# Gate and value products of a gated MLP as seven block products on tiles of 1024 tokens, with all attention scores ahead of the tiles

## Chip, cores and metric

The kernel runs on one core of one Trainium2 chip. The metric is the device time of one execution in microseconds; lower is better. Times of the kernel before are the median, lowest and highest of 3 runs, and one more execution was profiled.

## The reference

Everything is float32. The attention works over channels, the MLP over tokens.

```
B, N, C = 2, 6016, 256            # q, k, v: [B, N, C];  d_ff = 1536
qn = q / (norm(q, axis=1) + 1e-6);  kn = k / (norm(k, axis=1) + 1e-6)
s  = kn.transpose(0, 2, 1) @ qn / tau                 # [B, 256, 256]
a  = exp(s - max(s, -1));  a /= a.sum(-1) + 1e-9
x  = (v @ a).reshape(12032, 256)                      # tokens
xn = x / sqrt(mean(x * x, -1) + 1e-6) * rms_g
g  = xn @ w_gate;  val = xn @ w_val                   # [12032, 1536]
out = (g * sigmoid(g) * val) @ w_out                  # [12032, 256]
```

## The kernel before

**Arithmetic.** For precision every float32 operand of a large product is split in a high part (`_hi`, rounded by ScalarE to the matmul's format) and a low part (`_lo`, the rest, by VectorE), and a product is three matmuls: high by high, high by low, low by high (`product`, L382). So each 128x128 weight block costs three matmuls over a tile's columns. The scores of the first batch are made from unsplit float32 instead (`raw_scores`, L391).

**Stages.** A group is four chunks of 128 tokens of q and k (12 groups a batch, one of three chunks). SP loads groups into a ring of three buffers; TensorE makes the scores, ScalarE squares q and k for the norms, VectorE adds the squares up. All 12 groups of batch 0 and four of batch 1 pass so ahead of the tiles. Norms, softmax and the split of `a` follow for batch 0. The other eight groups of batch 1 pass during the first eight tiles, split in high and low (`scores1`, L404).

A tile is 512 tokens (12 a batch, one of 384). Of the next tile, v is loaded and turned by VectorE (`turn_v`), split (`vt`), multiplied with `a` (`attend`, L435), scaled by the inverse root of its mean square (`x_rms`, `x_scale`), passed through DRAM by SP (`pass_x`, L313), turned (`turn_x`) and split (`xt`), all between the units of the current tile.

**A unit** is one of 12 slices of 128 of d_ff. `gate_val` (L458) makes the gate (2 weight blocks, 6 matmuls, bank `ps_gate`) and the value (6 more, `ps_val`). ScalarE makes silu (L632), VectorE the product with the value (L882), ScalarE its high part (L636), VectorE its low part (L887). `project` (L470) then adds 2 blocks of 3 matmuls to the output banks `ps_out`, one unit behind:

```
gate_val(t, odd, f, n)
project(t, f - 1, n)
```

The units use two buffers in turn: TensorE waits for `hid_done` of two units ago before a gate and for `hid_split` before a projection. After unit 11 VectorE turns `ps_out` to `stage` (L1009) and SP stores it. The order on each engine is written out by hand in `step`. GpSimd only makes two constants.

## Time and profile before

| | us |
|---|---|
| median of 3 runs | 1343.12 (1339.2 to 1345.58) |
| profiled execution, own time | 1343.76 |
| its span | 1342.0 |
| TensorE busy | 1317.4 (98%), 6224 matmul records |
| VectorE busy | 701.6 (52%), 1294 instructions |
| ScalarE busy | 529.0 (39%), 1008 instructions |
| GpSimd busy | 0.8 (0%), 7 instructions |
| moved by DMA | 78.10 MB, mean 58 GB/s |
| mean granted TensorE clock | 0.992 |

The span is the profiled window on the core; the own time is what that execution took, 1.76 us more. The profile calls TensorE PE, VectorE DVE, ScalarE ACT, GpSimd POOL and SyncE SP. A busy time counts the instructions' own time only; matmuls overlap, so the mean of one is longer than the pace at which they follow each other, and the pace is what sums to time.

### The profile page before, as it was taken

The page shows a single profiled execution, that of the slowest core. Times are in us where ns is not written, and L with a number is a line of the kernel's source. Part 1 is how long each engine was busy: PE and PEld are TensorE (multiplying, and loading weights), DVE is VectorE, ACT ScalarE, POOL GpSimd, SP SyncE. Part 2 cuts the span into 40 slices and gives each one's busy share as a digit, 9 for nine tenths or more (in the row PEclk, how much of TensorE's full clock was granted, in tenths as well). Part 3 has the DMA queues.
Part 4 walks back from the last instruction along what each step waited for, and adds up shares of the span by engine and source line. Part 5 has one row for each costly group of instructions (what it writes and reads, how often), then busy time and mean ns, then how long its engine had stood idle before and what let it go on. Part 6 is the DMA issues. An engine that isn't in the chain of part 4 may idle for free.

```text
span 1342.0 us, 17895 instructions
## 1 busy us (share of the span) xinstructions
PE 1317.4 (98%) x6224; PEld 1117.1 (83%) x6224; DVE 701.6 (52%) x1294; ACT 529.0 (39%) x1008; POOL 0.8 (0%) x7
## 2 busy tenths in 40 slices
PE   8889999999999999999999999999999999999998
PEld 7768888888888888888888888888888888888887
DVE  4775555555555555455454455454454454454453
ACT  5564434344344343333343333333333333333332
POOL 0000000000000000000000000000000000000000
PEclk9899999999999999999999999999999999999999
DMA  8851212312223112111112111121121121121010
GB/s 295 274 153 47 63 32 72 84 31 63 50 68 70 31 31 63 32 28 46 42 32 55 36 32 36 43 46 31 32 62 31 31 63 31 31 59 32 16 40 12
DMA packets 171192, 78.10 MB, mean 58 GB/s; under 512 B 148626, under 2 KB 165010, under 8 KB 171154
## 3 DMA queue, kind: packets, MB, share of 16 engines
q1 hardware_dynamic: 171154, 77.62, 22.2%
q8 instruction: 21, 0.34, 0.1%
q14 instruction: 17, 0.14, 0.0%
HBM read 53.48 MB, written 24.12 MB: 58 GB/s over the span
## 4 chain that ended last, share of the span: by engine, by line
PE 94%; DVE 2%; DMA 2%; ACT 1%; issue 1%; SPq 0%; DVEq 0%; ACTq 0%
PE ps_out L387 28%; PE ps_gate L387 28%; PE ps_val L387 28%; PE ps_aux L387 7%; PE ps_aux L396 2%; DMA raw<-in_k_dram 1%; PE ps_out L396 1%; DVE hid L882 0%; ACT hid_hi L636 0%; DMA xn<-x_rows 0%; DVE hid_lo L887 0%; DMA x_rows<-xn 0%; DVE stage L1009 0%; DVE wo_lo L915 0%; ACT s_acc L585 0%
## 5 line engine op out<-in xcount | busy, mean ns | idle before, releaser
L882 DVE TENSOR_TENSOR hid<-ps_val,sg 128x512 f32<-128x512 f32 (+1 forms) x288 | 195.4, 679 | 349.5 <-PE ps_val L387 335.3
L636 ACT ACTIVATE hid_hi<-hid 128x512 fp32r<-128x512 f32 (+1 forms) x288 | 179.6, 624 | 457.5 <-DVE hid L882 457.5
L887 DVE TENSOR_TENSOR hid_lo<-hid,hid_hi 128x512 fp32r<-128x512 f32 (+1 forms) x288 | 196.2, 681 | 201.9 <-ACT hid_hi L636 201.9
L632 ACT ACTIVATE sg<-ps_gate 128x512 f32<-128x512 f32 (+1 forms) x288 | 169.8, 590 | 248.3 <-PE ps_gate L387 247.8
L387 PE MATMUL ps_out<-hid_hi,wo_hi 128*128 128x512 f32 (+1 forms) x576 | 222.8, 387 | 4.7 <-DVE hid_lo L887 4.3
L387 PE MATMUL ps_gate<-xt_hi,wgv_hi 128*128 128x512 f32 (+1 forms) x576 | 222.9, 387 | 2.1 <-DVE xt_lo L873 2.1
L387 PE MATMUL ps_gate<-xt_lo,wgv_hi 128*128 128x512 f32 (+1 forms) x576 | 222.2, 386 | 0.0
L387 PE MATMUL ps_out<-hid_hi,wo_lo 128*128 128x512 f32 (+1 forms) x576 | 222.0, 385 | 0.0
L387 PE MATMUL ps_out<-hid_lo,wo_hi 128*128 128x512 f32 (+1 forms) x576 | 221.8, 385 | 0.0
L387 PE MATMUL ps_gate<-xt_hi,wgv_lo 128*128 128x512 f32 (+1 forms) x576 | 221.8, 385 | 0.0
L387 PE MATMUL ps_val<-xt_hi,wgv_lo 128*128 128x512 f32 (+1 forms) x576 | 221.5, 384 | 0.0
L387 PE MATMUL ps_val<-xt_lo,wgv_hi 128*128 128x512 f32 (+1 forms) x576 | 221.5, 384 | 0.0
L387 PE MATMUL ps_val<-xt_hi,wgv_hi 128*128 128x512 f32 (+1 forms) x576 | 221.4, 384 | 0.0
L387 PEld LDWEIGHTS ps_out<-hid_hi,wo_hi 128*128 128x128 f32 x576 | 108.2, 188 | 29.0 <-DVE hid_lo L887 7.8
L387 PEld LDWEIGHTS ps_gate<-xt_hi,wgv_hi 128*128 128x128 f32 x576 | 108.4, 188 | 23.1 <-issue 2.1
L387 PEld LDWEIGHTS ps_gate<-xt_hi,wgv_lo 128*128 128x128 f32 x576 | 108.4, 188 | 21.0
L387 PEld LDWEIGHTS ps_out<-hid_hi,wo_lo 128*128 128x128 f32 x576 | 108.3, 188 | 20.7
L387 PEld LDWEIGHTS ps_val<-xt_hi,wgv_hi 128*128 128x128 f32 x576 | 108.1, 188 | 20.7
L387 PEld LDWEIGHTS ps_val<-xt_lo,wgv_hi 128*128 128x128 f32 x576 | 108.1, 188 | 20.7
L387 PEld LDWEIGHTS ps_val<-xt_hi,wgv_lo 128*128 128x128 f32 x576 | 108.1, 188 | 20.5
L387 PEld LDWEIGHTS ps_out<-hid_lo,wo_hi 128*128 128x128 f32 x576 | 108.3, 188 | 20.3
L387 PEld LDWEIGHTS ps_gate<-xt_lo,wgv_hi 128*128 128x128 f32 x576 | 108.5, 188 | 19.6
(100 smaller groups left out, 1030.6 us busy)
## 6 DMA issues: line engine op xcount, KB each, us to landing
v_in<-in_v_dram SPq DMA_DIRECT2D x88, 128.0 KB, 3.1
out_dram<-stage SPq DMA_DIRECT2D x88, 128.0 KB, 2.4
raw<-in_q_dram SPq DMA_DIRECT2D x21, 512.0 KB, 4.2
raw<-in_k_dram SPq DMA_DIRECT2D x21, 512.0 KB, 5.3
x_rows<-xn SPq DMA_DIRECT2D x21, 512.0 KB, 2.9
xn<-x_rows SPq DMA_DIRECT2D x84, 128.0 KB, 2.8
stage<-in_moe_w_out_dram SPq DMA_DIRECT2D x6, 256.0 KB, 3.2
raw<-in_q_dram SPq DMA_DIRECT2D x3, 384.0 KB, 4.6
```

What stands on the lines that cost most here:

```text
L387: last = nc.tensor.matmul(ps, lhs[h][a], rhs[h][c], start=start and h == 0 and m == 0, stop=stop and h == n - 1 and m == 2)
L396: last = nc.tensor.matmul(banks[c][:, 0:C], every_h(raw[:, r, 1, j * C:(j + 1) * C], c), raw[:, r, 0, j * C:(j + 1) * C], start=first and ...
L632: nc.scalar.activation(sg[:, s, 0:n * P], ps_gate[s][:, 0:n * P], ACT.Silu).then_inc(silu_done, 1)
L636: nc.scalar.activation(hid_hi[:, s, 0:n * P], hid[:, s, 0:n * P], ACT.Copy)\
L882: nc.vector.tensor_tensor(hid[:, s, 0:n * P], ps_val[s][:, 0:n * P], sg[:, s, 0:n * P], ALU.mult)\
L887: nc.vector.tensor_tensor(hid_lo[:, s, 0:n * P], hid[:, s, 0:n * P], fl(hid_hi[:, s, 0:n * P]), ALU.subtract).then_inc(hid_split, 1)
```

## The change

**Seven products for eight.** A tile is now 1024 tokens in two halves of 512 (12 tiles; the last has two halves of 384). A unit is 256 columns of d_ff, and for gate and for value the product is one of 2x2 blocks by 2x2 blocks: A, the weights, by the unit's two slices of 128 columns and the two halves of the channels; B, the tokens, by halves of the channels and halves of the tile. It is done by the seven-product scheme in the form with fifteen sums: P1 = A11 B11, P2 = A12 B21, P3 = S4 B22, P4 = A22 T4, P5 = S1 T1, P6 = S2 T2, P7 = S3 T3, where S1 to S4 are sums of weight blocks and T1 to T4 sums of token blocks. A phase (`phase`) makes the gate (m = 0) or the value (m = 1) of a unit: seven products of three matmuls in three banks `ps_r`, `ps_p`, `ps_q`. A later product adds onto what lies in a bank after another engine read the partial sum from there: ScalarE copies P1 (`snapshot`), VectorE makes u2, u3, c22, c21 and c12 by five additions of a bank to a buffer (`combine`), and `ps_r` itself becomes c11. The projection of the unit before (4 items of 2 blocks, 24 matmuls) stands between the products, 12 matmuls a phase, so that a phase is 33 matmuls.

**Work moved and added.** GpSimd now makes the weights' scaled and mixed blocks and their low parts (`scale_piece`, `mix_piece`, `piece_lo`, `wo_lo_piece`) ahead of the tiles, and in a unit the four low parts of the hidden items and two of the four gate-value multiplications. VectorE keeps the other two, the combinations, the turns, and forms the T blocks (`x_mix`) and their low parts (`late_low`). ScalarE gets a snapshot a phase, and copies x out of its bank (`x_squares`).

**All scores ahead.** All 24 groups of q and k pass as raw float32 before the first tile; `scores1` and the splits of q and k are gone. The loops are unrolled.

The core of the diff (removed and added functions, in the order TensorE, ScalarE, VectorE, GpSimd):

```diff
-            def gate_val(tile, slot, f, n, fresh=False):
-                U = NF * tile + f
-                if f == 0:
-                    pe.wait_ge(xt_done, tile + 1)
-                if not fresh:
-                    pe.wait_ge(hid_done, U - 1)
-                fs = slice(f * P, (f + 1) * P)
-                rhs = [(xt_hi[:, slot, h, 0:n * P], xt_lo[:, slot, h, 0:n * P]) for h in range(H)]
-                for s, (ps, done) in enumerate(((ps_gate, gate_mm), (ps_val, val_mm))):
-                    product(ps[f % 2][:, 0:n * P], [(wgv_hi[:, h, s, fs], wgv_lo[:, h, s, fs]) for h in range(H)],
-                            rhs, True, True).then_inc(done, 1)
+            def multiply(ps, s, u, m, w, x, start=False):
+                n = width(s)
+                slot = x_slot(s, x)
+                return passes(ps[:, 0:n * P], (wc_hi[:, u, w, m, :], wc_lo[:, u, w, m, :]),
+                              (xo_hi[:, slot, 0:n * P], xo_lo[:, slot, 0:n * P]), start, True, goes_on=not start)
+            def phase(s, u, m):
+                G = UNITS * s + u
+                q = 2 * G + m
+                fresh = u == 0 and m == 0
+                if fresh:
+                    pe.wait_ge(x_split, 2 * s + 1)
+                if s == 0 and m == 0:
+                    pe.wait_ge(wpiece, u + 1)
+                if m:
+                    pe.wait_ge(silu_done, 4 * G + 1)
+                elif G > 0:
+                    pe.wait_ge(h11_done, G)
+                multiply(ps_r, s, u, m, A11, B11, start=True).then_inc(p1_mm, 1)
+
+                if q > 0:
+                    pe.wait_ge(c21_done, q)
+                if fresh:
+                    pe.wait_ge(late_split, 5 * s + 1)
+                multiply(ps_p, s, u, m, S2, T2, start=True).then_inc(p6_mm, 1)
+
+                if G > 0:
+                    project(G - 1, 2 * m, 0)
+
+                if q > 0:
+                    pe.wait_ge(c12_done, q)
+                if fresh:
+                    pe.wait_ge(late_split, 5 * s + 2)
+                multiply(ps_q, s, u, m, S1, T1, start=True)
+
+                if fresh:
+                    pe.wait_ge(x_split, 2 * s + 2)
+                pe.wait_ge(s1_done, q + 1)
+                multiply(ps_r, s, u, m, A12, B21).then_inc(p2_mm, 1)
+
+                if fresh:
+                    pe.wait_ge(late_split, 5 * s + 3)
+                pe.wait_ge(u2_done, q + 1)
+                multiply(ps_p, s, u, m, S3, T3).then_inc(p7_mm, 1)
+
+                if G > 0:
+                    project(G - 1, 2 * m, 1)
+                    project(G - 1, 2 * m + 1, 0)
+
+                if fresh:
+                    pe.wait_ge(late_split, 5 * s + 4)
+                pe.wait_ge(u3_done, q + 1)
+                multiply(ps_p, s, u, m, A22, T4).then_inc(p4_mm, 1)
+
+                if G > 0:
+                    project(G - 1, 2 * m + 1, 1)
+
+                if fresh:
+                    pe.wait_ge(late_split, 5 * s + 5)
+                pe.wait_ge(c22_done, q + 1)
+                multiply(ps_q, s, u, m, S4, B22).then_inc(p3_mm, 1)
...
+            for G in range(GROUPS):
+                raw_scores(G)
+            raw_scores(GROUPS)
+            pe.wait_ge(consts, 2)
+            pe.wait_ge(tau_in, 16)
+            norms(0, ps_r)
+            raw_scores(GROUPS + 1)
+            spread(0, ps_r)
+            for G in range(GROUPS + 2, GROUPS + 5):
+                raw_scores(G)
+            pe.wait_ge(a_done, 1)
+            for piece in range(4):
+                attend(0, piece, first_banks[piece]).then_inc(x_mm, 1)
+                G, j = GROUPS + 5 + piece // 2, piece % 2 * 2
+                raw_scores(G, j, j + 2)
+            for G in (GROUPS + 7, GROUPS + 8):
+                raw_scores(G)
+            turn_x0(0)
+            raw_scores(GROUPS + 9)
+            turn_x0(1)
+            for G in (GROUPS + 10, GROUPS + 11):
+                raw_scores(G)
+            pe.wait_ge(x_turned, 2)
...
+            def snapshot(q, dst):
+                w = P * width(q // PHASES)
+                act.wait_ge(p1_mm, q + 1)
+                nc.scalar.activation(dst[:, 0:w], ps_r[:, 0:w], ACT.Copy).then_inc(s1_done, 1)
+
+            def silu(G, dst, src, ready):
+                w = P * width(G // UNITS)
+                act.wait_ge(ready, 2 * G + 1)
+                nc.scalar.activation(dst[:, 0:w], src[:, 0:w], ACT.Silu).then_inc(silu_done, 1)
...
-            def unit(tile, f, n, fresh=False):
-                U = NF * tile + f
-                s = f % 2
-                dve.wait_ge(silu_done, U + 1)
-                dve.wait_ge(val_mm, U + 1)
-                nc.vector.tensor_tensor(hid[:, s, 0:n * P], ps_val[s][:, 0:n * P], sg[:, s, 0:n * P], ALU.mult)\
-                    .then_inc(hid_done, 1)
-                dve.wait_ge(hid_hi_done, U + 1)
-                if not fresh:
-                    dve.wait_ge(out_mm, U - 1)
-                nc.vector.tensor_tensor(hid_lo[:, s, 0:n * P], hid[:, s, 0:n * P], fl(hid_hi[:, s, 0:n * P]),
-                                        ALU.subtract).then_inc(hid_split, 1)
+            def combine(q, dst, src, bank, ready, done):
+                w = P * width(q // PHASES)
+                dve.wait_ge(ready, q + 1)
+                nc.vector.tensor_tensor(dst[:, 0:w], src[:, 0:w], bank[:, 0:w], ALU.add).then_inc(done, 1)
...
+                    q = 2 * G + 1
+                    sg11, sg12 = c11, u2
+                    s1, u2, u3, c11 = (vs[:, i, :] for i in range(4))
+                    if G > 0:
+                        dve.wait_ge(hid_split, 4 * G)
+                    combine(q, u2, s1, ps_p, p6_mm, u2_done)
+                    if more and u == 1:
+                        vt_low(s + 1, 1)
+                    if more and u == 2:
+                        vt_low(s + 1, 3)
+                    if more and u == 5:
+                        late_low(s + 1, T2)
+                    dve.wait_ge(p2_mm, q + 1)
+                    dve.wait_ge(silu_done, 4 * G + 1)
+                    nc.vector.tensor_tensor(c11[:, 0:w], sg11[:, 0:w], ps_r[:, 0:w], ALU.mult).then_inc(h11_done, 1)
+                    combine(q, u3, s1, ps_p, p7_mm, u3_done)
+                    combine(q, u3, u3, ps_q, u3_done, c22_done)
+                    if s > 0 and u == 0:
...
+                    if more and u == 4:
+                        x_mix(s + 1, 0)
...
+                    combine(q, s1, s1, ps_p, p4_mm, c21_done)
...
+                    combine(q, u2, u2, ps_q, p3_mm, c12_done)
+                    dve.wait_ge(c12_done, q + 1)
+                    dve.wait_ge(silu_done, 4 * G + 4)
+                    nc.vector.tensor_tensor(u2[:, 0:w], u2[:, 0:w], sg12[:, 0:w], ALU.mult).then_inc(mul12_done, 1)
...
+            def mix_piece(u):
+                a11, a12, a21, a22 = (gv_block(u % 2, h, half) for half in range(2) for h in range(2))
+                s1, s2, s3, s4 = (mixed_block(i) for i in range(4))
+                if u > 0:
+                    pool.wait_ge(wpiece, u)
+                nc.gpsimd.tensor_tensor(s3, a11, a21, ALU.subtract)
+                chain(nc.gpsimd.tensor_tensor(s1, a21, a22, ALU.add))
+                chain(nc.gpsimd.tensor_tensor(s2, s1, a11, ALU.subtract))
+                nc.gpsimd.tensor_tensor(s4, a12, s2, ALU.subtract).then_inc(mixed_done, 1)
+
+            def piece_lo(u):
+                pool.wait_ge(wpiece_hi, u + 1)
+                for i, (h, half) in enumerate(((0, 0), (1, 0), (1, 1))):
+                    nc.gpsimd.tensor_tensor(wc_lo[:, u, i, :, :], gv_block(u % 2, h, half),
+                                            fl(wc_hi[:, u, i, :, :]), ALU.subtract)
+                nc.gpsimd.tensor_tensor(wc_lo[:, u, 3:7, :, :].rearrange("p i s f -> p (i s f)"), mixed[:, :],
+                                        fl(wc_hi[:, u, 3:7, :, :].rearrange("p i s f -> p (i s f)")),
+                                        ALU.subtract).then_inc(wpiece, 1)
...
+            def hid_low(G, item, src):
+                w = P * width(G // UNITS)
+                pool.wait_ge(hid_hi_done, 4 * G + item + 1)
+                nc.gpsimd.tensor_tensor(hid_lo[:, item, 0:w], src[:, 0:w], fl(hid_hi[:, item, 0:w]), ALU.subtract)\
+                    .then_inc(hid_split, 1)
+
+            def multiply(G, item, val, gate, val_done):
+                w = P * width(G // UNITS)
+                pool.wait_ge(val_done, 2 * G + 2)
+                pool.wait_ge(silu_done, 4 * G + item + 1)
+                nc.gpsimd.tensor_tensor(val[:, 0:w], val[:, 0:w], gate[:, 0:w], ALU.mult).then_inc(mul_done, 1)
...
```

How the rows stand on the engines. TensorE, before, in the middle of a tile: the end of one projection and the next gate (the number after a bank's name is its buffer).

```order
L387 MATMUL ps_out1<-hid_hi,wo_hi 128x512
L387 MATMUL ps_out1<-hid_lo,wo_hi 128x512
L387 MATMUL ps_out1<-hid_hi,wo_lo 128x512
L387 MATMUL ps_gate0<-xt_hi,wgv_hi 128x512 [waits hid_done]
L387 MATMUL ps_gate0<-xt_lo,wgv_hi 128x512
L387 MATMUL ps_gate0<-xt_hi,wgv_lo 128x512
```

TensorE, of the change, in a phase of tile 1, from the product P7 on:

```order
L461 MATMUL ps_p<-xo_hi,wc_hi 128x512 [waits u2_done]
L461 MATMUL ps_p<-xo_lo,wc_hi 128x512
L461 MATMUL ps_p<-xo_hi,wc_lo 128x512
L461 MATMUL ps_out10<-hid_hi,wo_hi 128x512
L461 MATMUL ps_out10<-hid_lo,wo_hi 128x512
L461 MATMUL ps_out10<-hid_hi,wo_lo 128x512
L461 MATMUL ps_out01<-hid_hi,wo_hi 128x512 [waits staged,hid_split]
L461 MATMUL ps_out01<-hid_lo,wo_hi 128x512
L461 MATMUL ps_out01<-hid_hi,wo_lo 128x512
L461 MATMUL ps_p<-xo_hi,wc_hi 128x512 [waits u3_done]
L461 MATMUL ps_p<-xo_lo,wc_hi 128x512
L461 MATMUL ps_p<-xo_hi,wc_lo 128x512
```

Where a bank was left alone until the unit was over, six matmuls now stand between the end of P7 and P4, which goes to the same bank and waits for `u3_done`, VectorE's read of it.

VectorE, before, at the end of a tile (two units and the turn of the output):

```order
L882 TENSOR_TENSOR hid<-ps_val,sg 128x512 [waits val_mm,silu_done]
L887 TENSOR_TENSOR hid_lo<-hid,hid_hi 128x512 [waits out_mm,hid_hi_done]
L1007 ISA [waits out_mm]
L1009 STREAM_TRANSPOSE stage<-ps_out 128x16x32 [waits slot_dma0]
L1009 STREAM_TRANSPOSE stage<-ps_out 128x16x32
```

VectorE, of the change, in the second phase (m = 1) of a tile's first unit:

```order
L1034 TENSOR_TENSOR vs<-vs,ps_p 128x512 [waits p6_mm,s1_done,hid_split]
L1136 TENSOR_TENSOR vs<-gs,ps_r 128x512 [waits silu_done,p2_mm]
L1034 TENSOR_TENSOR vs<-vs,ps_p 128x512 [waits p7_mm]
L1034 TENSOR_TENSOR vs<-vs,ps_q 128x512 [waits u3_done]
L1025 STREAM_TRANSPOSE out_t_58<-ps_out 128x16x32 [waits out_mm]
L1034 TENSOR_TENSOR vs<-vs,ps_p 128x512 [waits p4_mm]
L1025 STREAM_TRANSPOSE out_t_58<-ps_out 128x16x32
L1034 TENSOR_TENSOR vs<-vs,ps_q 128x512 [waits p3_mm]
L1171 TENSOR_TENSOR vs<-vs,gs 128x512 [waits silu_done,c12_done]
L976 TENSOR_TENSOR vt_lo<-xf,vt_hi 128x512 [waits vt_hi_done]
```

Seven instructions of the unit and three of the tile's own work stand in one phase, and five of the seven are waited for by TensorE within the phase or the next.

GpSimd, of the change, at the first tile (before, it has nothing after the constants):

```order
L404 TENSOR_TENSOR xo_lo<-xf,xo_hi 128x512 [waits x_hi_done,wpiece]
L404 TENSOR_TENSOR xo_lo<-xf,xo_hi 128x512 [waits x_hi_done]
L410 TENSOR_TENSOR hid_lo<-vs,hid_hi 128x512 [waits hid_hi_done,acc_done]
L417 TENSOR_TENSOR vs<-vs,gs 128x512 [waits silu_done,c22_done]
L417 TENSOR_TENSOR vs<-vs,gs 128x512 [waits silu_done,c21_done]
L410 TENSOR_TENSOR hid_lo<-vs,hid_hi 128x512 [waits hid_hi_done] x4
```

The first row is behind the last weight piece (`wpiece`), and TensorE's first product of the first tile waits for it (`x_split`); from then on it is six instructions a unit, four low parts and two multiplications.

## Rows read from the trace of the kernel before

**Rows 1.** The page, busy times and the 40 slices (33.6 us each).

```profile
PE 1317.4 (98%) x6224; PEld 1117.1 (83%) x6224; DVE 701.6 (52%) x1294; ACT 529.0 (39%) x1008; POOL 0.8 (0%) x7
...
PE   8889999999999999999999999999999999999998
...
PEclk9899999999999999999999999999999999999999
```

**Rows 2.** Windows: start and end, length, busy per engine, clock, DMA share, GB/s.

```profile
20.00:40.00 20.00, 19.33 (x90) 17.24 (x89) 14.80 (x16) 13.25 (x16) 0.00 (x0) 1.00 0.96 345
...
60.00:80.00 20.00, 16.06 (x74) 14.09 (x73) 13.50 (x35) 9.20 (x24) 0.00 (x0) 0.86 0.33 107
...
250.00:500.00 250.00, 250.00 (x1206) 211.04 (x1205) 137.14 (x234) 103.83 (x195) 0.00 (x0) 1.00 0.23 55
```

**Rows 3.** Chain of waits in a tile: start, length, what.

```profile
600.45 2.87 PE ps_aux L387 x24
603.32 1.39 PE ps_gate L387 x6
604.71 1.36 PE ps_val L387 x6
606.07 1.36 PE ps_out L387 x6
```

**Rows 4.** Chain of waits from the start to the first tile.

```profile
6.13 18.17 PE ps_aux L396 x72
...
24.92 6.90 DMA raw<-in_k_dram
...
84.02 1.63 PE ps_gate L387 x6
```

**Rows 5.** Timeline of PE ahead of the tiles: start, length, instructions.

```profile
65.22 3.63 PE L396 MATMUL ps_out<-raw 128*128 128x256 f32 x16
...
80.23 1.20 PE L454 MATMUL ps_aux<-ident,xn 128*128 128x128 f32 x8 [1.73 <-DVE xn L857]
```

**Rows 6.** Groups of instructions by line and shape: count, busy, mean ns, idle before.

```profile
L882 DVE TENSOR_TENSOR hid<-ps_val,sg 128x512 f32<-128x512 f32 x264 | 182.1, 690 | 324.7 <-PE ps_val L387 310.5 <-ACT sg L632 11.9 <-DVE rinv L769 1.7
L636 ACT ACTIVATE hid_hi<-hid 128x512 fp32r<-128x512 f32 x264 | 166.9, 632 | 424.3 <-DVE hid L882 424.3
L747 DVE TENSOR_TENSOR sqr_acc<-sqr_acc,sqr 128x1024 f32<-128x1024 f32 x40 | 47.9, 1220 | 10.1 <-ACT sqr L563 10.1
L563 ACT ACTIVATE sqr<-raw 128x1024 f32<-128x1024 f32 x40 | 40.8, 1049 | 13.4 <-DMA raw<-in_k_dram 13.4
L857 DVE TENSOR_SCALAR xn<-ps_aux,rinv 128x256 f32<-128x256 f32 x46 | 20.1, 478 | 0.0
```

**Rows 7.** The same view, GpSimd alone.

```profile
L376 POOL TENSOR_SCALAR_AFFINE_SELECT ident<-ident 128x128 f32<-128x128 f32 x1 | 0.3, 294 | 0.1
...
L1030 POOL MEMSET const-float32-0.0<- 128x1 f32 x1 | 0.1, 99 | 0.2 <-issue 0.2
```

**Rows 8.** Timeline of PE at one late low part.

```profile
102.06 0.39 PE L387 MATMUL ps_val<-xt_hi,wgv_lo 128*128 128x512 f32 x1
102.72 0.50 PE L387 MATMUL ps_out<-hid_hi,wo_hi 128*128 128x512 f32 x1 [0.27 <-DVE hid_lo L887]
103.06 0.39 PE L387 MATMUL ps_out<-hid_lo,wo_hi 128*128 128x512 f32 x1
```

**Rows 9.** Timeline of SP at one pass of x through DRAM.

```profile
342.56 0.39 SPq L317 DMA_DIRECT2D x_rows<-xn  x1
345.51 1.91 SPq L320 DMA_DIRECT2D xn<-x_rows  x4
```

**Rows 10.** Chain of waits at the end.

```profile
1331.45 1.04 PE ps_gate L387 x6
...
1333.64 0.57 DVE hid L882
...
1337.35 0.47 DVEq L53
```

More of the change, by code:

```diff
@@ L265, in wo_piece @@
                 half = WO_CHUNKS // 2
                 for s in range(2):
[L267 to L275 removed]
+                    at = WO_CHUNKS * piece + s * half
@@ L380, in _ @@
+            finish(UNITS * TILES - 1)
         @block.tensor
         def _(pe):
[L382 to L389 removed]
@@ L557, in _ @@
+            G = UNITS * TILES - 1
+            for item in range(4):
+                for c in range(H):
+                    project(G, item, c)
         @block.scalar
         def _(act):
-            def squares(G, w, slot, n, free=None, out=sqr):
-                if free is not None:
-                    act.wait_ge(acc_done, free)
-                nc.scalar.activation(out[:, w, 0:n * C], raw[:, slot, w, 0:n * C], ACT.Square)\
-                    .then_inc(sq_done, 1)
-            def freed(G, w):
-                return adds(G - 2) + w + 1
@@ L962, in step @@
[L962 to L978 removed]
+                add_squares(GROUPS + 9 + half)
@@ L988, in step @@
+                    if s == 2 and u == 0:
                         row_sums(1)
[L989 to L1003 removed]
@@ L1020 @@
+                    if more and u == 4:
+                        x_mix(s + 1, 2)
+            for half in range(2):
+                for c in range(H):
+                    turn_out(TILES - 1, half, c)
 _INS = ['q', 'k', 'v', 'tau', 'moe_w_gate', 'moe_w_val', 'moe_w_out', 'moe_rms_g']
```

1288 lines of the change are left out of this document (680 added, 608 removed).

## The prediction

> **What bounds the kernel now.** I read the page first: TensorE is busy 98% of the span, VectorE half of it, GpSimd nothing, and the clock is below full only early [rows 1]. Then the windows: from 250 to 500 us TensorE has no idle time at all, at full clock, with VectorE at 55% and ScalarE at 42%; only the stretch ahead of the tiles differs, where DMA runs at 345 GB/s (0.96 of its share) from 20 to 40 us and at a third of that from 60 to 80, with TensorE below full [rows 2]. The chain of waits inside a tile is nothing but matmuls: six of 512 columns in 1.36 us, 24 of 256 columns (`attend`) in 2.87 [rows 3]. So in the tiles time is the number of matmuls times their pace, 0.227 us, and it falls with their number as long as no other engine comes late. Ahead of them the chain goes over raw scores and loads until the first gate at 84.0 us [rows 4].
>
> **Matmuls of the tiles.** Before: a unit of 512 tokens is 18 matmuls, a tile 216 = 36 sixes. 22 full tiles x 36 x 1.36 [rows 3] = 1077.1 us; two short ones x 36 x 1.04 [rows 10] = 74.9; attends of tiles 1 to 23, 21 x 2.87 + 2 x 2.15 = 64.6; eight `scores1` of 24 matmuls x 2.87 = 23.0. Sum 1239.6. With the start at 84.0 that gives 1323.6 of the span's 1342.0; the other 18.4 are about 8 of tail, from the end of the last value product (1333.5 [rows 10]) to 1342.0, and 11 of small waits.
>
> After: gate and value of 1024 tokens x 256 columns cost 2 x 7 x 3 = 42 matmuls where they cost 48; the projection stays at 24. A tile is 6 x 66 = 396 matmuls = 66 sixes. 11 x 66 x 1.36 = 987.4; the last, 66 x 1.04 = 68.6; attends, 10 x 2 x 2.87 + 4.3 = 61.7; no `scores1`. Sum **1117.7, or 121.9 less**. The order of the matmuls confirms the counts (4356 of 512 columns, 396 of 384).
>
> **Ahead of the tiles.** A raw group is 16 records in 3.63 us [rows 5] (a float32 matmul leaves two), against 2.87 for a split one: moving eight groups costs TensorE 6 us on balance, but now all 23.5 full groups stand ahead: 23.5 x 3.63 = 85.3. With the attends of tile 0 (5.7), the turn of x (2 x 1.2 [rows 5]) and norms and spread (2.5) it is 96 us of TensorE from 6.1 us on [rows 4]: the first tile can't start before **102**. DMA needs less: 24.6 MB of q and k, 3.1 of weights, 1.1 of v, 0.5 of w_out, 29.4 MB at 345 GB/s [rows 2] = 85 us, from 2 us on. ScalarE (23 x 2.1 [rows 6] + 29 of other work) and VectorE (23 x 2.44 [rows 6]) would fit.
>
> GpSimd may not. Its work has no row before; the nearest are a one-input select on 128 elements, 0.294 us, and a fill of one, 0.099 [rows 7]: 1.5 ns an element, so 0.88 us for 512, with one input. Two inputs can't cost less than VectorE's 0.69 [rows 6], and at twice the select's rate per element they are 1.66. I take **1.2**, the middle. A weight piece is then 2 x 0.88 + 7 of 256 (0.65) + one of 1024 (2.3) = 8.6 us; six are 52, six `wo_lo` 7, two `x_lo` 2.4: 61 us from about 15 us on, with waits for ScalarE's high parts 82 us, just inside the 102. But VectorE adds squares meanwhile, 55 us of instructions with both inputs in SBUF. If the two exclude each other, it is 15 + 61 + 55 = 131 us. The Trainium skill says so ("SBUF — State Buffer", Who interferes with whom): a VectorE instruction with two SBUF inputs and a GpSimd instruction that reads SBUF lock each other out for a whole instruction. By it the first tile would start at 131 and not 102; no row of before shows it. It would also price a GpSimd `tensor_tensor` at about 1.1 us for 512 ("GPSIMD Engine Reference", Performance versus the Vector engine: half the speed of VectorE). I take **112**, nearer to the unlocked end, because the additions come in pairs with pauses between (VectorE 14.8 of 20 us [rows 2]) that GpSimd can use: 28 us later than now.
>
> **A phase.** 33 matmuls are 7.49 us. Where each read of a bank falls, from a phase's start, with 0.26 us from the last matmul's start of its slot to the reader, and 0.69 a read [rows 6]:
> - P6 ends at 1.36; u2 is 1.62 to 2.31; P7 wants it at 3.41. Slack 1.1.
> - P7 ends at 4.09; u3 is 4.35 to 5.04; P4 wants it at 5.45. Slack **0.4**, the least.
> - c22 is 5.04 to 5.73, P3 wants it at 6.81. c21 and c12 end at 7.08 and 8.44 and are wanted at 8.17 and 9.53, in the next phase. Slack 1.1 each.
>
> ScalarE's snapshot (0.63) is 0.94 to 1.57, wanted at 2.72. So in the plain phase nothing is late. In a value phase c11 (at 3.67, after P2) ends at 4.36, just before u3. The tile's own work fills the gaps: a turn, a low part or a mix of 0.69 each, x_scale of 4 x 0.48 [rows 6] after c22, the 12 short instructions of x_rms (2.4 us) before or after c12 with an attend (1.44) as cover. A value phase with three of these (units 3, 4 and 5) has 4.8 + 3 x 0.69 = 6.9 us or more of 7.5 and ends u2 of the next phase at about 10.6 where 10.9 is wanted. VectorE in all: 12 x 0.69 a unit, x 6, + 25 of tile work = 75 of 95.5 us a tile, 78%. A late read costs what it is late plus a refill: the late low part before left 0.66 us between two starts, and 0.34 to the next, for 0.227 [rows 8].
>
> GpSimd in a unit: 6 x 1.2 = 7.2 of 15 us. The tightest: it multiplies items 1 and 2 after the value's c22 and c21 (5.73 and 7.08), then makes item 1's low part, there at about 9.5; the projection wants it 21 matmuls into the next phase, at 12.3. That holds up to about 2 us an instruction.
>
> x's pass through DRAM: store issued, 2.95 us later the four loads, 1.9 to issue and some 2.8 to land [rows 9] make 7.4 us; the second half's x_scale ends at 7.7 of a phase and its turn is due 7 us later: near, a wait of up to 0.5 once a tile.
>
> What an exclusion would do in the tiles: one multiplication a unit and 13 low parts and mixes a tile have both inputs in SBUF; each could wait up to 1.2 us where GpSimd is busy (half the time), but with slack near 1 only part reaches TensorE. Bounds for all waits of TensorE in the tiles: as before, 11 less the early ones, so about 8, and 4 us a tile, 48 plus those 8 to 10. I take **23**, plus 3 to fill the first unit, which has no projection between its products.
>
> **Tail.** After P3 now come c12, multiplication, high part on ScalarE, low part on GpSimd, projection of the last item, turn, store: one instruction more, while items 0 to 2 project meanwhile. 7, as before within 1.
>
> **Sum.** 112 + 1117.7 + 3 + 23 + 7 = 1262.7 of span, + 1.8 to the own time = **1265**. The profiled execution (1343.76) lies 0.6 above the median of the runs, which I leave. Against before: -121.9 of matmuls, +28 at the start, +15 of waits and filling.
>
> **Rivals.**
> - *Smooth*: no lock, GpSimd near VectorE's pace. 103 + 1117.7 + 3 + 8 + 7 + 1.8 = **1241**. For it: every slack above is positive. Against: VectorE at 78% with a strict order. Chance 0.27.
> - *Forecast*, part of it: 1252 to 1285. Chance 0.38.
> - *Lock in both places*: 131 + 1117.7 + 3 + 50 + 7 + 1.8 = **1311**. For it: ahead of the tiles both engines have over 55 us of work on the same memory in some 80 us. Against: the pauses between VectorE's pairs. Chance 0.25.
> - *Slower, GpSimd and VectorE as one engine*: if every VectorE instruction, those with a bank as input too, shut GpSimd out, a unit would take 12 x 0.69 + 25 / 6 + 7.2 = 19.7 us where TensorE needs 15.9. Then 11.75 tiles x 6 x 19.7 + 131 + 12 = **1532**. It decides from (1350 - 131 - 12) / 70.5 = 17.1 us a unit; a GpSimd instruction of 2.85 us would do it alone. Against it stands that twice the select's rate gives 1.66. Chance 0.06, with 0.04 left for what lies between 1335 and 1350.
> - That the products aren't saved is excluded by the order of the matmuls. That adding onto a bank that was read costs more than 0.227 would show in the pace; in before `ps_out` takes sixes spread over a tile at 1.36 [rows 3], so I give it nothing of its own.
>
> **Chances.** A measurement of this kernel tells about 0.5% from no change. Faster: 0.27 + 0.38 + 0.25 + half of the 0.04 = 0.92; same the other half, 0.02; slower 0.06. Range 1236 to 1318: it leaves out the lower edge of the smooth case (0.05), the upper of the locked (0.06) and the slower ones (0.08).
>
> **What would show it.** Right: 396 matmuls a tile at 1.36 a six; the first P1 near 112, waiting for `xo_lo` of GpSimd; tiles 97 to 98 us apart; small waits of PE on u3 and c12 in units 3 to 5. Smooth: start near 103, tiles at 96. Locked: start beyond 125, additions of squares and `mul12` much longer than 1.22 and 0.69, tiles near 100. Wrong altogether: GpSimd at over 90% in the tiles, or a pace above 0.24.

## The result, and the profile after

The changed kernel takes **1377.07 us** (median of 4 runs, 1375.19 to 1381.36), the kernel before 1342.61 on the same chip. The ratio is 1.0262, with a 95% interval of 1.0227 to 1.0297: **slower by 2.6%**, where 1265 was predicted and 1318 was the upper end. The profiled execution has a span of 1374.6 us and a mean clock of 0.981.

The page of the changed kernel, against [rows 1]: busy times, then TensorE and its clock in 40 slices of 34.4 us.

```profile
PE 1266.7 (92%) x5736; PEld 1038.2 (76%) x5736; DVE 1057.3 (77%) x1652; ACT 623.1 (45%) x1186; POOL 743.3 (54%) x529
...
PE   8678698899899999999999999999999999999997
...
PEclk9889898999999999999999999999999999999999
```

TensorE is at 92% where it was at 98%: 50.7 us less of busy time, in a span that is 32.6 longer. Ahead of the first product of the tiles it is busy 38 us more than before, from there on 88 us less. VectorE is up by half, GpSimd is at 54%. The windows of the changed kernel, with the columns of [rows 2]:

```profile
20.00:40.00 20.00, 19.67 (x90) 16.91 (x89) 12.39 (x8) 10.11 (x12) 19.60 (x13) 1.00 0.68 247
40.00:60.00 20.00, 12.57 (x47) 10.35 (x45) 13.20 (x8) 8.09 (x10) 19.52 (x14) 0.83 0.88 234
...
250.00:500.00 250.00, 236.06 (x1063) 189.64 (x1064) 201.94 (x317) 114.52 (x220) 131.60 (x90) 1.00 0.17 39
```

From 20 to 60 us it is GpSimd that works without a break; DMA is at 0.68 of its share where it was at 0.96; in the tiles TensorE is idle for 14 of 250 us at full clock. TensorE's timeline at the first products of the tiles:

```profile
145.93 0.77 PE L461 MATMUL ps_r<-xo_hi,wc_hi 128*128 128x512 f32 x1 [6.37 <-issue]
150.43 0.80 PE L461 MATMUL ps_p<-xo_hi,wc_hi 128*128 128x512 f32 x1 [2.89 <-DVE xo_lo L1018]
```

The first tile starts at **145.9**, not at 112. Less 1117.7 of matmuls and about 7 of tail, 1374.6 - 145.9 leaves 104 us of waits and filling in the tiles, where 26 were in the sum. These two are the miss: +34 and +78, together 112 of the 1377 - 1265.

GpSimd at the end of the start (timeline; in brackets the idle time before):

```profile
123.31 2.10 POOL L386 TENSOR_TENSOR wc_lo<-gs,wc_hi 128x256 fp32r<-128x256 f32 x3 [13.52 <-ACT wc_hi L678]
...
144.56 2.49 POOL L404 TENSOR_TENSOR xo_lo<-xf,xo_hi 128x512 fp32r<-128x512 f32 x2
```

The first product of the tiles starts when the first of these two low parts of x ends, as the prediction had it. GpSimd's last weight piece had waited 13.5 us for its high part by ScalarE.

**A tile by units.** I take the times of ScalarE's copy of P1 of each value phase (`vs<-ps_r`, 72 of them) and average the distance to the next over tiles 1 to 10. From unit 0's to unit 1's and from 2's to 3's stand 66 matmuls and one attend, which are 66 x 0.227 + 1.43 = 16.4 us; from 1's to 2's two attends, 17.8; the other three, 66 matmuls alone, 15.0.

| from the value phase of unit | 0 | 1 | 2 | 3 | 4 | 5 | tile |
|---|---|---|---|---|---|---|---|
| matmuls alone | 16.4 | 17.8 | 16.4 | 15.0 | 15.0 | 15.0 | 95.5 |
| changed kernel | 17.44 | 17.89 | 16.75 | 16.91 | 16.81 | 16.66 | 102.5 |
| a1_pool_writes | 16.41 | 17.81 | 16.60 | 16.34 | 14.98 | 15.01 | 97.2 |
| a2_pool_short | 16.41 | 17.81 | 16.75 | 15.62 | 14.96 | 15.01 | 96.6 |
| a3_scale_on_act | 17.44 | 17.89 | 16.81 | 15.65 | 16.78 | 16.67 | 101.2 |
| c1_mix_short | 17.45 | 17.89 | 16.75 | 16.89 | 15.45 | 14.97 | 99.4 |
| d1_two_buffers | 17.44 | 17.89 | 16.74 | 15.62 | 16.81 | 16.65 | 101.2 |
| e2_order_alone | 16.41 | 17.89 | 16.73 | 16.90 | 14.96 | 15.88 | 98.8 |
| f2_order_and_writes | 16.41 | 17.81 | 16.60 | 16.34 | 14.96 | 15.01 | 97.1 |
| e1_order_and_rest | 16.41 | 17.89 | 16.75 | 15.63 | 14.96 | 15.87 | 97.5 |

Seven us a tile are lost, nearly all in four places: 1.0, 1.9, 1.8 and 1.7 us after units 0, 3, 4 and 5. Tile 0 takes 115.7, 20 more than its matmuls (104.8 in a1, 101.0 in a2).

**What stands at such a place.** VectorE, then GpSimd, then TensorE of the changed kernel at the end of unit 4 of a tile (timeline: start, length, instruction; in brackets the idle time before it):

```profile
557.92 0.67 DVE L1034 TENSOR_TENSOR vs<-vs,ps_q 128x512 f32<-128x512 f32 x1
558.62 1.08 DVE L1171 TENSOR_TENSOR vs<-vs,gs 128x512 f32<-128x512 f32 x1
559.62 1.77 DVE L1008 TENSOR_TENSOR t<-xf 128x512 f32<-128x512 f32 x1
561.32 0.67 DVE L1034 TENSOR_TENSOR gs<-gs,ps_p 128x512 f32<-128x512 f32 x1
561.92 1.16 DVE L1012 TENSOR_TENSOR xf<-xf,t 128x512 f32<-128x512 f32 x1
```

```profile
559.11 5.12 POOL L410 TENSOR_TENSOR hid_lo<-vs,hid_hi 128x512 fp32r<-128x512 f32 x3
```

```profile
560.41 0.39 PE L461 MATMUL ps_r<-xo_hi,wc_lo 128*128 128x512 f32 x1
562.05 0.50 PE L461 MATMUL ps_p<-xo_hi,wc_hi 128*128 128x512 f32 x1 [1.25 <-DVE gs L1034]
```

The sums that read a bank (L1034) take 0.67 us, as the evictions did [rows 6]. The mixings, with both inputs in SBUF, take 1.77 and 1.16 beside GpSimd's three low parts. The one of 1.77 stands ahead of the sum u2 (561.32), which TensorE needs for P7: it waits 1.25 us. The groups of the changed kernel from 250 to 1300 us show how large this is (columns of [rows 6]; L1171 is `mul12`, VectorE's multiplication at the end of a unit, L993 the scaling of x, L1018 the late low parts):

```profile
L1171 DVE TENSOR_TENSOR vs<-vs,gs 128x512 f32<-128x512 f32 x61 | 62.2, 1020 | 2.1
L993 DVE TENSOR_SCALAR io<-io,rinv 128x256 f32<-128x256 f32 x78 | 51.6, 720 | 0.0
...
L1018 DVE TENSOR_TENSOR xo_lo<-xf,xo_hi 128x512 fp32r<-128x512 f32 x40 | 50.3, 1277 | 0.0
```

```profile
L410 POOL TENSOR_TENSOR hid_lo<-vs,hid_hi 128x512 fp32r<-128x512 f32 x246 | 368.1, 1513 | 454.9 <-ACT hid_hi L761 454.5
```

### The profile page after: what moved, and what is told of

The parts are those of the page before. It is cut to its first block, busy times and chain, and to the rows that moved or that the text cites. A ratio compares the mean times of both kernels' runs of the same rounds, so it can differ in the third digit from the quotient of the medians.

```text
span 1374.6 us, 16549 instructions
## 1 busy us (share of the span) xinstructions
PE 1266.7 (92%) x5736; PEld 1038.2 (76%) x5736; DVE 1057.3 (77%) x1652; ACT 623.1 (45%) x1186; POOL 743.3 (54%) x529
## 4 chain that ended last, share of the span: by engine, by line
PE 35%; POOL 28%; issue 20%; DVE 14%; ACT 2%; DMA 1%; SPq 0%; DVEq 0%; POOLq 0%; ACTq 0%
POOL hid_lo L410 13%; PE ps_out L461 10%; POOL vs L417 9%; PE ps_p L461 8%; PE ps_r L461 5%; PE ps_q L461 5%; PE ps_x L461 4%; DVE vs L1034 2%; POOL xo_lo L404 2%; DVE gs L1034 2%; DVE io L993 2%; DVE vt_lo L976 2%; PE ps_out L475 1%; DVE sqr_acc L871 1%; DVE vs L1136 1%
## 5 line engine op out<-in xcount | busy, mean ns | idle before, releaser
L410 POOL TENSOR_TENSOR hid_lo<-vs,hid_hi 128x512 fp32r<-128x512 f32 (+1 forms) x288 | 419.7, 1475 | 543.3 <-ACT hid_hi L761 542.7
L761 ACT ACTIVATE hid_hi<-vs 128x512 fp32r<-128x512 f32 (+1 forms) x288 | 173.1, 618 | 261.2 <-POOL vs L417 172.2
L461 PE MATMUL ps_p<-xo_hi,wc_hi 128*128 128x512 f32 (+1 forms) x432 | 175.3, 406 | 52.3 <-DVE gs L1034 39.0
L1034 DVE TENSOR_TENSOR gs<-gs,ps_p 128x512 f32<-128x512 f32 (+1 forms) x216 | 144.6, 670 | 99.8 <-PE ps_p L461 91.9
L417 POOL TENSOR_TENSOR vs<-vs,gs 128x512 f32<-128x512 f32 (+1 forms) x144 | 202.2, 1419 | 34.0 <-DVE vs L1034 34.0
L754 ACT ACTIVATE gs<-gs 128x512 f32<-128x512 f32 (+1 forms) x216 | 134.1, 621 | 179.2 <-DVE gs L1034 176.5
L1034 DVE TENSOR_TENSOR vs<-vs,ps_p 128x512 f32<-128x512 f32 (+1 forms) x216 | 145.0, 671 | 42.1 <-PE ps_p L461 26.4
L461 PE MATMUL ps_p<-xo_lo,wc_hi 128*128 128x512 f32 (+1 forms) x432 | 167.8, 389 | 0.0
L461 PE MATMUL ps_p<-xo_hi,wc_lo 128*128 128x512 f32 (+1 forms) x432 | 167.5, 388 | 0.0
L461 PE MATMUL ps_r<-xo_hi,wc_hi 128*128 128x512 f32 (+1 forms) x288 | 114.1, 396 | 8.6 <-issue 6.4
L1034 DVE TENSOR_TENSOR gs<-gs,ps_q 128x512 f32<-128x512 f32 (+1 forms) x144 | 97.0, 674 | 22.9 <-PE ps_q L461 18.8
```

The lines of the kernel that those rows point to most:

```text
L410: nc.gpsimd.tensor_tensor(hid_lo[:, item, 0:w], src[:, 0:w], fl(hid_hi[:, item, 0:w]), ALU.subtract)\
L417: nc.gpsimd.tensor_tensor(val[:, 0:w], val[:, 0:w], gate[:, 0:w], ALU.mult).then_inc(mul_done, 1)
L461: last = nc.tensor.matmul(ps, lhs[a], rhs[c], start=start and i == 0, stop=stop and i == 2, skip_group_check=goes_on)
L754: nc.scalar.activation(dst[:, 0:w], src[:, 0:w], ACT.Silu).then_inc(silu_done, 1)
L761: nc.scalar.activation(hid_hi[:, item, 0:w], src[:, 0:w], ACT.Copy).then_inc(hid_hi_done, 1)
L1034: nc.vector.tensor_tensor(dst[:, 0:w], src[:, 0:w], bank[:, 0:w], ALU.add).then_inc(done, 1)
```

## The experiments

All start from the changed kernel unless a line says otherwise. Times with a ratio are medians of several runs; the others are one run each. a1, a2, a4, c1, f1 and f2 leave work out or write constants in its place, so their outputs are not the reference's.

**a1 and a2: GpSimd's work in the tiles.**

```
a1, and the multiplication likewise (two fills of 0.53 us for each instruction):
-  nc.gpsimd.tensor_tensor(hid_lo[:, item, 0:w], src[:, 0:w], fl(hid_hi[:, item, 0:w]), ALU.subtract)
+  chain(nc.gpsimd.memset(fl(hid_lo[:, item, 0:w]), 0.25))
+  nc.gpsimd.memset(fl(hid_lo[:, item, 0:w]), 0.25)
a2, in both:
+  w = w if G == 0 else 8
```

> GpSimd's six instructions of a unit only write now: two fills of a constant for each (some 0.5 us apiece), so it stays busy about as long and is as late, but reads nothing; the hidden items and their low parts are constants. Theory lock (a GpSimd instruction that reads SBUF and a VectorE instruction with two SBUF inputs exclude each other): the multiplication of item 3 falls from 1.03 to 0.69 us, the low parts and mixes from 1.1 to 1.7 to 0.69, TensorE's waits in the tiles from about 98 to 50 to 80 us, total 1330 to 1360. Rival length (GpSimd is simply slow and late): these durations and the total stay, 1370 to 1380.

> GpSimd's six instructions of a unit work on 8 columns instead of 512 after the first unit; most of the low parts and of two of the four multiplications is left out. Neither lock nor lateness of GpSimd is left in the tiles. Theory lock: x_scale, low parts, mixes back to VectorE's own durations, waits of TensorE in the tiles from 98 to 25 to 45 us, total 1310 to 1330. Rival order (VectorE's own order and load make the waits, at 77%): waits stay above 70, total 1350 or more.

Measured: a1 1309.83, a2 1301.0. The first product stays where it was. So 67 us go when GpSimd still works 562.6 us (of 743.3) but reads nothing in a unit's six instructions, and only 9 more when it hardly works, at 242.4 us. The same groups of a1:

```profile
L1172 DVE TENSOR_TENSOR vs<-vs,gs 128x512 f32<-128x512 f32 x61 | 42.2, 692 | 2.1
L1019 DVE TENSOR_TENSOR xo_lo<-xf,xo_hi 128x512 fp32r<-128x512 f32 x40 | 26.6, 684 | 0.0
```

0.69 where it was 1.02 and 1.28. So it is exclusion: an instruction of the one engine waits for one of the other. It costs more than I expected: both times lie below the ranges that I gave. One thing a1 doesn't separate: its two fills (1.06 us) are also shorter than an undisturbed instruction of GpSimd (1.29), so some of the 67 us can be that GpSimd is done earlier. e2 below keeps GpSimd's instructions as they are.

**a3: x_scale on ScalarE.**

```
-  last = nc.vector.tensor_scalar(part, part, rinv[...], None, ALU.mult)
+  last = nc.scalar.activation(part, part, ACT.Copy, scale=rinv[...])
```

> The scaling of x by the inverse root, 8 instructions of 0.69 us a tile on VectorE, goes to ScalarE (46 to 48% busy), the result is the same. If VectorE's queue in units 3 to 5 makes the waits: 1 to 2 us less a tile, total 1355 to 1368. If not, within 3 us of 1377.

Measured: 1359.62, ratio to before 1.014 (1.0114 to 1.0167). It is 17 us less than the changed kernel, as the theory had it. The table says where: in the full tiles after unit 3 alone, 1.3 of its 1.9 us.

**a4: the additions of squares on 8 columns.**

```
-  nc.vector.tensor_tensor(acc, acc, sqr[:, w, 0:n * C], ALU.add)
+  nc.vector.tensor_tensor(acc[:, 0:8], acc[:, 0:8], sqr[:, w, 0:8], ALU.add)
```

> VectorE's additions of squares work on 8 columns instead of 1024; the norms are wrong thereby. Theory lock: GpSimd's instructions on a weight piece fall to their own durations, 0.73 us for 256 columns against 1.66 beside the additions, its cycle of one piece from 16.4 to 11 or 12 us, and the first tile starts at 120 to 130 instead of 146: total 1350 to 1360. Rival length (GpSimd's own work, and ScalarE waiting for it): the cycle stays above 14 us and the start at 138 or later.

Measured: 1353.38; the first product at 127.1, 19 us earlier; tiles 1 to 10 are as they were (102.4), tile 0 takes 3 less. GpSimd's groups from 20 to 130 us, first of the changed kernel, then of a4:

```profile
L386 POOL TENSOR_TENSOR wc_lo<-gs,wc_hi 128x256 fp32r<-128x256 f32 x18 | 22.6, 1284 | 13.9 <-ACT wc_hi L678 13.5
L369 POOL TENSOR_SCALAR gs<-gs,gcol 128x512 f32<-128x512 f32 x12 | 22.4, 1878 | 24.0 <-DMA gs<-in_moe_w_val_dram 24.0
```

```profile
L369 POOL TENSOR_SCALAR gs<-gs,gcol 128x512 f32<-128x512 f32 x12 | 19.0, 1597 | 28.6 <-DMA gs<-in_moe_w_val_dram 28.6
...
L386 POOL TENSOR_TENSOR wc_lo<-gs,wc_hi 128x256 fp32r<-128x256 f32 x18 | 12.6, 730 | 16.4 <-ACT wc_hi L678 16.0
...
L396 POOL TENSOR_TENSOR wo_lo<-gs,wo_hi 128x512 fp32r<-128x512 f32 x4 | 5.1, 1292 | 6.8 <-ACT wo_hi L685 6.8
```

**f1: GpSimd's work ahead of the tiles as memsets** (the mixtures and low parts are constants, the scaling is left out).

```
-  nc.gpsimd.tensor_tensor(wc_lo[:, u, 3:7, :, :]..., mixed[:, :], fl(wc_hi[:, u, 3:7, :, :]...), ALU.subtract)
+  nc.gpsimd.memset(fl(wc_lo[:, u, :, :, :]...), 0.0)
```

> The changed kernel, with GpSimd's work ahead of the tiles (scalings, mixtures, low parts of the weights and of the first tile's x) replaced by memsets that read nothing from SBUF; all waits stay. The low parts are zero and the mixtures a constant, so the output is not the reference's. Theory 1 (GpSimd's time for the weights, lock included, sets the start, as b1 and d2 leave possible): the first product starts at 105 to 120 instead of 145.9, the time is 1337 to 1352, and VectorE's additions of squares take 1.2 us instead of 1.9. Theory 2 (the queues of the pass, each in the order written, and its transfers set it): the first product starts above 130 and the time stays above 1360.

Measured: 1350.97, the first product at 120.6, VectorE's additions at 1.22 us where they were at 1.59. This is the other half of the same pair: 25 of the 34 us at the start are GpSimd's time and its exclusion with the additions together; f1 takes both away and can't part them. 8.6 above my 112 remain.

**b1: the scaling of the weights on ScalarE (the pieces' high parts move one group later with it); b2: b1 and a3 together.**

```
-  last = nc.gpsimd.tensor_scalar(part[:, h, :, :], part[:, h, :, :], gcol[:, h:h + 1], None, ALU.mult)
+  last = nc.scalar.activation(part[:, h, :, :], part[:, h, :, :], ACT.Copy, scale=gcol[:, h:h + 1])
```

> GpSimd's cycle for a weight piece was 16.4 us here, two scalings of 3.1 us together among it, and ScalarE is idle for most of the pass. The scaling by the gains goes to ScalarE. Theory 1 (the start is set by GpSimd's chain of weight pieces, ended by its output-weight low parts): the cycle falls to 12 or 13 us, the first product starts 10 to 20 us earlier, at 125 to 135 instead of 145.9, and the time falls to 1355 to 1367. Theory 2 (the start is set by the stream of squares, raw scores and DMAs, and GpSimd only ends last): the first product moves by less than 4 us and the time stays above 1372.

> The weight pieces' scaling and the scaling of x both on ScalarE. Theory: the two act in different places (before the first product, and in the tiles), so their gains add: 17 us for x, 10 to 20 for the weights, 1339 to 1350, about level with the kernel before (1340). Rival: one of the two is hidden by the other (ScalarE's queue becomes late for hi parts): 1355 or above.

Measured: b1 1372.34, b2 1358.71 (ratio to before 1.0116, 1.0096 to 1.0137). Theory 2 held in b1: GpSimd loses 22 us of work and the first product comes 3 us earlier (142.8). In b2 the rival held, with 1 us on top of a3. The time freed on GpSimd turned into waits between queues: GpSimd waits 67 us for ScalarE ahead of the tiles, where it waited 20. TensorE's waits ahead of the tiles in b1:

```profile
PE ps_r L451 <- issue: 7.5, 1, 7.5
PE ps_x L451 <- DVE vt_lo L977: 7.0, 1, 7.0
PE ps_r L451 <- DVE vt_lo L977: 5.0, 1, 5.0
PE ps_p L451 <- DVE vt_lo L977: 4.2, 1, 4.2
```

In the changed kernel the first is 6.4, and those for `vt_lo` are 6.6, 4.0, 1.6 and 1.6.

**c1: mixings and late low parts of x on 8 columns from tile 1 on.**

```
-  w = P * width(s)
+  w = P * width(s) if s == 0 else 8
```

> From the second tile on, VectorE's four x mixings and five late low parts of a tile run on 8 columns only (their partial sums of x are left stale, so the output is not the reference's). They are 9 instructions of 1.1 to 1.7 us in units 3 to 5 and 0 of the tile, 121 us in all. Theory 1 (the waits of TensorE in the tiles sit where VectorE's queue is overfull, in units 4 and 5, and the GpSimd lock only pushes it over): TensorE's waits for VectorE's sums of the gates (39 us now) fall to under 12 and the time to 1325 or below. Theory 2 (the lock costs the same everywhere, by each collision on the critical additions): the waits stay above 25 and the time at 1355 or above.

Measured: 1342.57, waits for sums of the gates 18.2 us where they were 39.0. This lies between both theories. It gives 34 us, in the full tiles all of it after units 4 and 5; the 1.0 after unit 0 and the 1.9 after unit 3 are untouched. So the loss has places, and each place its own instruction; that asked for the next readings.

**d1: a second buffer for S1 and c21 of the gates in odd units, from the third tile on** (b2 with this), so that ScalarE's copy needn't wait for GpSimd's product of the unit before.

```
-  act.wait_ge(mul_done, 2 * G)
+  act.wait_ge(mul_done, 2 * (G if G < SPLIT else G - 1))
```

> b2_both_on_act, and the buffer that holds S1 and then the sum c21 of the gates gets a second copy for odd units from the third tile on, so that ScalarE's copy of S1 of a unit no longer waits for GpSimd's last multiplication of the unit before. Theory 1 (the lock reaches TensorE through one chain: VectorE's c21, GpSimd's product, ScalarE's copy into the same buffer, VectorE's next sum, TensorE's S3 product; it costs 0.7 us in each unit, where 2.04 us of TensorE's work cover 1.9 us unlocked and 2.4 or more locked): 59 units lose up to 0.7 us each, the time is 1322 to 1340, and the unit without other work falls from 15.7 to under 15.2. Theory 2 (VectorE's own stretched instructions delay its sums, wherever GpSimd's result is wanted): 15.7 stays, and the time is above 1350.

Measured: 1357.06 against 1358.71, and no unit of the table moves. My theory fell. The chain through GpSimd is real: ScalarE's copies into that buffer waited for GpSimd 61 times in b2, 57.0 us in all, and 10 times in d1, 15.1 us. But VectorE took its place: at the end of unit 4 its next sum stands behind a mixing of 1.8 us in either kernel, and TensorE waits 1.6 us for that sum in d1 where it waited 1.25 in b2.

**d2: the start in another order** (from d1).

```
 if G == GROUPS + 5:
+    vt_high(0, 1)
     x_squares(0, 0, first_banks[0])
-    vt_high(0, 1)
...
+            vt_low(0, 3)
             x_rms(0, 0)
             x_scale(0, 0)
-            vt_low(0, 3)
```

> d1_two_buffers, and the start written in another order: ScalarE takes the high parts of v ahead of the copies of x, scales and splits the sixth weight piece as soon as it is there, VectorE takes the last low part of v ahead of the inverse roots, and the last output weights are fetched a group earlier. No instruction is added or removed. Theory 1 (what holds the start is the order in the queues, each of which waits for the next: TensorE waits 7.0, 4.2 and 5.0 us for low parts of v, and the sixth piece waits 13.7 us for ScalarE with its mixtures ready): the first product starts 8 to 20 us earlier than 143, the time is 8 to 20 us under d1_two_buffers. Theory 2 (the transfers of the pass set the start): under 4 us.

Measured: 1351.17 (ratio 1.006, 1.004 to 1.0079), the first product at 136.4 where it was at 141.4. The gain of 5.9 us lies between the theories: the order counts, for less than I thought. (The order of the transfers is part of it: the last output weights are fetched a group earlier.)

**e2: seven of VectorE's instructions in a tile moved (the expectation miscounts them as eight); e1: the same moves in d2.** Nothing is added or taken away:

```
 unit 0, gate:   late_low(s, B22)        from behind u2        to behind c22
 unit 0, end:    turn_out(s - 1, 1, 0)   from unit 1's gate    to here
 unit 1, gate:   vt_low(s + 1, 0)        from unit 0's end     to behind c22
 unit 4, value:  x_mix(s + 1, 0)         from behind c22       to behind u2
 unit 5, gate:   x_mix(s + 1, 1)         from unit 4's value   to behind c22
 unit 5, gate:   x_mix(s + 1, 2)         from unit 4's end     to behind c21
 unit 5, gate:   x_mix(s + 1, 3)         from behind u2        to behind c12
```

> The changed kernel with eight of VectorE's instructions in a tile moved to other places of its queue and nothing else changed: the four mixings of x, the last late low part, the first low part of v and one output transposition. Before, they stood right behind the products of a unit or ahead of the first sums of the next, where GpSimd works without a break on three low parts of 1.3 us, and a VectorE instruction with two inputs in SBUF took 1.2 to 1.8 us; now they stand behind the gates' sums, where GpSimd is idle for 7 us, or ahead of its first low part. Theory 1 (what TensorE loses in a tile is a locked VectorE instruction of 1.2 to 2.8 us that stands ahead of a sum it waits for; by place: 1.0 us from unit 0 to 1, 1.8 from 4 to 5, 1.7 from 5 to 0): up to 4 us a tile go, 11 tiles, the time falls by 30 to 44, to 1333 to 1347, and VectorE's mixings take about 0.7 us again. Theory 2 (the lock costs by the amount of overlapping work, wherever it stands): the time falls by less than 10.

> The same moves in d2_start_order (1351). Theory 1: the same 30 to 44 us, to 1307 to 1321, which is under the kernel before (1342). Theory 2: above 1341.

Measured: **e2 1335.66** (10 runs, ratio to before 0.9959, 0.9944 to 0.9973), **e1 1309.98** (ratio 0.9773, 0.9747 to 0.9799). The moves give 41 us in either kernel, as theory 1 had it; but in e1 3.9 of the 41 are a start that came earlier than in d2, for which the moves are no reason. By the table it is 3.7 us a tile in either. The losses after units 0 and 4 are gone whole, 0.8 of the 1.7 after unit 5. The timeline of VectorE in e2 where unit 5 begins, to hold against the one above:

```profile
549.18 0.69 DVE L1034 TENSOR_TENSOR gs<-gs,ps_q 128x512 f32<-128x512 f32 x1
549.78 0.68 DVE L1006 TENSOR_TENSOR xf<-xf 128x512 f32<-128x512 f32 x1
550.50 0.69 DVE L1034 TENSOR_TENSOR gs<-gs,ps_p 128x512 f32<-128x512 f32 x1
551.10 0.69 DVE L1008 TENSOR_TENSOR t<-xf 128x512 f32<-128x512 f32 x1
551.86 0.69 DVE L1034 TENSOR_TENSOR gs<-gs,ps_q 128x512 f32<-128x512 f32 x1
552.46 0.69 DVE L1012 TENSOR_TENSOR xf<-xf,t 128x512 f32<-128x512 f32 x1
```

The same mixings take 0.69. Over the whole of e1, which is faster than the kernel before by 2.3%, the page says:

```profile
PE 1244.4 (95%) x5736; PEld 1040.1 (80%) x5736; DVE 954.5 (73%) x1558; ACT 668.8 (51%) x1292; POOL 689.2 (53%) x517
```

Part of what is left after unit 5 is my own mistake of the same kind: I put the late low part of B22 behind c22 in the belief that GpSimd was done by then. In e2 it wasn't:

```profile
565.24 1.37 DVE L1018 TENSOR_TENSOR xo_lo<-xf,xo_hi 128x512 fp32r<-128x512 f32 x1
566.53 0.68 DVE L1034 TENSOR_TENSOR gs<-gs,ps_p 128x512 f32<-128x512 f32 x1
```

P3, which needs this low part, starts at 566.66 and is 0.3 us late by it. Another 0.5 of the 0.9 is lost at P2 of the same phase (562.17): ScalarE's copy of P1 had waited 1.07 us for GpSimd's product.

**f2: e2's order with a1's memsets.**

> e2_order_alone (1335.7), and GpSimd's six instructions of a unit replaced by memsets of the same length as in a1_pool_writes (1309.8). The output is not the reference's. If the moves did their work by taking locked VectorE instructions from the places where sums are due, little is left of the lock: 1303 to 1320, and e2_order_alone lies 15 to 30 us above it, most of that in the unit from 5 to 0 and in the starts of units. If the moves shortened the queue in general, both gains add: under 1295.

Measured: 1312.63, a tile of 97.12 us against 97.15 in a1 (1309.83; the first product comes 3.1 us later here, which is the difference). Where GpSimd only writes, the order is worth nothing; where it reads, 3.7 us a tile. With e2's mixings at 0.69 this shows that the moves work by the exclusion, and not by a shorter queue.

## Why the prediction was wrong, point by point

- **Number and pace of the matmuls: right.** 66 matmuls without other work take 14.96 us where the tiles are undisturbed, 0.227 each; so 121.9 us are saved. TensorE's waits and the later start gave them back.
- **GpSimd at 1.2 us an instruction: slightly low.** Undisturbed it is 1.29 for two inputs of 512 columns. But one-input scaling, taken at 0.88, is 1.6, and 256 columns are 0.73 instead of 0.65. A weight piece is so 10.7 us and not 8.6 (2 x 1.60 + 7 x 0.73 + 2.37, from the rows of a4), before any exclusion.
- **The start at 112: failed, the first term of the sum.** I wrote that the pauses between VectorE's pairs of additions could be used by GpSimd, and went to the unlocked end. They are hardly worth anything: GpSimd comes round every 16.4 us from 28 to 61 us, for a piece that takes 10.7 undisturbed, while six additions (7.3) pass; one after the other the two would be 18.0. An addition lengthens from 1.22 to 1.59 us in the mean (34 of 1024 columns up to 130 us), GpSimd's 256 columns from 0.73 to 1.28. a4 and f1 price GpSimd's part at 19 to 25 us. Even the fully locked 131 was too low, because a second term was missing: from 88 us on GpSimd stands idle for 5.8 us (a load of weights), 13.5 and 6.6 (ScalarE's high parts), where the sum had some 6 us of such waits in all. ScalarE, VectorE, SP and TensorE pass the squares and v through queues written in one order, so that a wait of one can become a wait of the next; d2 takes 6 us away by another order alone. That this makes up all of the rest is not shown.
- **"4 us a tile" as the upper bound of waits: failed, the second term of the sum.** It was 7.0, and 20 in tile 0. The step that failed is the one on exclusion: "with slack near 1 only part reaches TensorE". I priced locked instructions one by one against the slack of 1.1. But they stand two and three in a row ahead of a sum, exactly where GpSimd has three low parts in a row: `mul12` at 1.08, then a mixing at 1.77, are 1.5 us beyond the 1.38 that they take undisturbed, more than the slack. Exclusion in the tiles is worth up to 67 us by a1, and 41 by the moves of e2 alone.
- **Tile 0: no term held it.** 11 of its 20 us go in a1 and 15 in a2. Its largest wait, 6.5 us for the first sum of a gate, comes from the short instructions for the norms of batch 1, which stand ahead of that sum while GpSimd works without a pause. That wait is 4.3 us in a1 and under 1 in a2. One of these instructions, on 4 columns, takes 1.18 us beside GpSimd, and 0.16 once GpSimd has finished:

```profile
225.65 1.18 DVE L889 TENSOR_TENSOR nw<-nw 128x4 f32<-128x4 f32 x1
...
229.30 0.16 DVE L889 TENSOR_TENSOR nw<-nw 128x4 f32<-128x4 f32 x1
```

- **x_scale at 4 x 0.48, from a row that read PSUM [rows 6]: failed.** From SBUF four of them take 1.13 us where GpSimd hardly works (a2) and 2.68 beside GpSimd's reads, as in most tiles, against the 1.92 of the sum: the operation is quicker than I had it, and excluded too. It costs 1.3 us a tile after unit 3 (a3).
- **The rivals.** *Lock in both places* named the mechanism and both places, and its signs (start beyond 125, mul12 and additions longer, tiles near 100) all came, the tiles at 102.5. Its sizes, 131 and 50, were short by 15 and 51, so its 1311 was far off as well. *GpSimd and VectorE as one engine* did not come: sums that read a bank keep their 0.68, GpSimd is at 54%.
- **The choice between them.** The Trainium skill ("SBUF — State Buffer", Who interferes with whom) has a VectorE instruction with two SBUF inputs and a GpSimd instruction that reads SBUF shut each other out, and one that only writes doesn't. The trace agrees: 1.02 to 1.77 us beside reads, 0.69 beside memsets. I gave this rule 0.25 because no row of before showed it; a row could not, since GpSimd did nothing then.
- **Small slips, none of which carries the miss.** The loads ahead of the tiles count 0.5 MB of w_out, but the first product stands behind the low parts of all 1.6 MB: 88 us of DMA and not 85, still under 102. The parts of the pass through DRAM add up to 7.65 us, not 7.4. The upper bound of the waits is 56 to 58 us by its own parts, where the locked rival takes 50.

## What to carry to other kernels

When a change wakes an engine that was idle, the trace of before can't show what it disturbs. List for each instruction whether both engines use SBUF at once, and lay the two queues side by side: what counts is which locked instructions stand in a row ahead of a result that TensorE waits for. Then move those to where the other engine pauses; here this alone was worth 41 us, more than handing work to ScalarE (17 us in a3, 5 in b1). It brought the change from 2.6% slower to level with the kernel before, and together with a3, b1, d1 and d2 to 2.3% faster.
